# Two-path attention with two feed-forward layers on one core: band tiles of 26 queries by 32 keys in place of 58 by 64

## The reference

```
q_d, k_d, v_d = means over groups of 4 positions           # 144 rows each
out_up   = repeat(softmax(q_d k_d^T / 8) v_d, 4)            # the average path
scores   = q k^T / 8, where |i - j| < 4, else -1e9          # the band path: 7 keys a query
out_local = softmax(scores) v
x = out_up + out_local                                      # then (2304 tokens, 512)
x = (h * sigmoid(h)) @ w_out,        h = x @ w_in           # layer 1, 512 -> 2048 -> 512
x = (h * sigmoid(1.702 h)) @ w_out,  h = x @ w_in           # layer 2
```

## Time and profile before

| | |
|---|---|
| median of three runs | 809.04 us (807.85 to 809.33) |
| profiled execution | 808.21 us, span 806.4 us |
| TensorE, VectorE, ScalarE, GpSimd busy in the span | 98%, 80%, 66%, 26% |
| attention | from 5.3 us to 106.7 us |
| granted TensorE clock | full in every slice |

### The profile page before, as it was taken

One profiled execution on the slowest core, in us unless ns is written; L12 is line 12 of the kernel. 1 busy time (PEld: TensorE's weight loads), 2 busy tenths in 40 slices (PEclk: granted clock), 3 DMA queues, 4 the chain that ended last, 5 costly groups with the idle time before them and its releaser, 6 DMA issues.

```text
span 806.4 us, 15771 instructions
## 1 busy us (share of the span) xinstructions
PE 790.0 (98%) x5864; PEld 763.4 (95%) x5864; DVE 646.0 (80%) x905; ACT 530.8 (66%) x849; POOL 208.8 (26%) x203
## 2 busy tenths in 40 slices
PE   9888799999999999999999999999999999999998
PEld 5666599999999999999999999999999999999998
DVE  7999899999898778998678898899555688456466
ACT  5878865677655678555687556678455786465673
POOL 5899977520274220445200000000000000000000
PEclk9999999999999999999999999999999999999999
DMA  8877647787878887677877778868887877878773
GB/s 282 266 249 238 197 150 259 262 298 233 283 236 268 260 315 245 217 261 258 289 267 249 239 250 262 256 224 272 306 275 257 273 249 266 304 250 271 264 256 136
DMA packets 100763, 205.51 MB, mean 255 GB/s; under 512 B 8784, under 2 KB 56400, under 8 KB 100688
## 3 DMA queue, kind: packets, MB, share of 16 engines
q1 hardware_dynamic: 100688, 204.51, 76.0%
HBM read 160.96 MB, written 43.52 MB: 254 GB/s over the span
## 4 chain that ended last, share of the span: by engine, by line
PE 88%; POOL 8%; issue 3%; DVE 1%; ACT 0%; POOLq 0%; DVEq 0%
PE hid L351 43%; PE yp L377 42%; POOL vpair L1038 2%; POOL vavg L1042 1%; PE yp L393 1%; POOL pband L1032 1%; POOL G L1062 1%; POOL G L1063 1%; POOL G L1068 1%; POOL G L1066 1%; POOL x L284 0%; DVE wh L315 0%; PE sc L1342 0%; PE hp L1342 0%; PE pt L1229 0%
## 5 line engine op out<-in xcount | busy, mean ns | idle before, releaser
L351 PE MATMUL hid<-xs,wh 128*128 128x384 f32 x2016 | 351.3, 334 | 0.7 <-issue 0.4
L351 PEld LDWEIGHTS hid<-xs,wh 128*128 128x128 f32 x2016 | 349.3, 188 | 1.7 <-issue 1.4
L377 PE MATMUL yp<-gr,wh 128*128 128x384 f32 x1968 | 342.1, 334 | 0.0
L377 PEld LDWEIGHTS yp<-gr,wh 128*128 128x128 f32 x1968 | 341.2, 188 | 0.1
L306 ACT ACTIVATE wh<-wr 128x1024 fp32r<-128x1024 f32 (+1 forms) x164 | 164.6, 1004 | 149.8 <-PE hid L351 120.0
L569 DVE TENSOR_TENSOR gr<-G,gr 128x768 fp32r<-128x768 f32 x144 | 137.9, 964 | 52.7 <-ACT gr L449 52.7
L449 ACT ACTIVATE gr<-G 128x768 fp32r<-128x768 f32 x144 | 121.8, 845 | 66.9 <-PE yp L377 66.8
L315 DVE TENSOR_TENSOR wh<-wr,wh 128x1024 fp32r<-128x1024 f32 x76 | 95.1, 1251 | 19.0 <-ACT wh L306 18.8
L412 ACT ACTIVATE G<-G 128x1152 f32<-128x1152 f32 x48 | 55.7, 1161 | 0.8 <-DVE G L564 0.8
L533 DVE TENSOR_TENSOR hv<-p,hid 128x384 f32<-128x384 f32 x48 | 26.3, 548 | 29.8 <-PE hid L351 28.0
L559 DVE TENSOR_TENSOR G<-hv,hid 128x384 f32<-128x384 f32 x48 | 26.3, 549 | 28.2 <-PE hid L351 28.2
(11 more groups left out here) (101 smaller groups left out, 748.0 us busy)
## 6 DMA issues: line engine op xcount, KB each, us to landing
wh<-rests SPq DMA_DIRECT2D x72, 512.0 KB, 3.7
wr<-sums_out SPq DMA_DIRECT2D x48, 512.0 KB, 4.7
wr<-in_w_out SPq DMA_DIRECT2D x36, 512.0 KB, 5.2
rests<-wh SPq DMA_DIRECT2D x36, 512.0 KB, 3.5
wr<-sums_in SPq DMA_DIRECT2D x40, 384.0 KB, 4.0
wr<-in_w_in SPq DMA_DIRECT2D x40, 256.0 KB, 3.5
qk<-in_qkT SPq DMA_DIRECT2D x11, 576.0 KB, 4.8
G<-in_w_in SPq DMA_DIRECT2D x12, 512.0 KB, 5.3
```

The lines of the kernel that those rows point to most:

```text
L351: last = eng.matmul(hid[:, at, 0:HALF], lhsT=wh[:, w % SLOTS, part, a % 4, cc * P:(cc + 1) * P], rhs=xs[:, rest, q, cc, :], start=start an ...
L377: last = eng.matmul(yp[:, at + m, 0:HALF], lhsT=wh[:, w % SLOTS, part, p % 4, m * P:(m + 1) * P], rhs=gr[:, p, rest, :], start=start and p ...
```

## The change

22 tiles of 26 queries and 32 keys take the place of the 10 (the first and the last have 28 queries). In `scores` a slot is now 32 columns wide and holds four tiles, one on each 32 rows; 12 slots, 384 columns, head 0 in the first 192 and head 1 in the other 192, each in its own half of `sc`. The tiles of each head form two parts of 11.

- Scores: 44 matmuls (2 heads x 22 tiles), weights 64 features by 32 queries, 32 moving columns; for each tile head 0, then head 1. The outer tiles are no exception any more, and the wait on `half_sc` is gone.
- Mask: two bf16 products of 192 columns. It is made by more steps: GpSimd fills `band4` and `ends` and cuts them with six affine selects, VectorE takes a maximum over four (new semaphore `band_max`), and ScalarE copies in three steps.
- VectorE's three passes and ScalarE's exponential go over 12 slots of 32 columns (33 with a guard); GpSimd's multiplication writes to a tile of its own, `probs`, in another order, so VectorE's subtraction has a new wait on `b_nrm` of two units back.
- Transposes: three of 128x128 in one group, where there were five in two; one copy of 384 columns where there were two. There are three groups a unit in place of four.
- Band products: 44 matmuls, weights 32 keys by 64 features, 26 moving columns (28 at the ends). The keys of (head, part) = (0,0), (0,1), (1,0), (1,1) lie on rows 0, 32, 64 and 96 onwards. Part 0 writes the first half of `po`, part 1 the second; head h writes output rows 64h onwards. `vwin` holds 11 windows of 64 features on each row, where it had 5 of 128.

```diff
-    QT = 64
-    WIN = 64
-    NT = 10
-    HALF = NT // 2
+    QT = 32
+    WIN = 32
+    PART = 11
+    NT = 2 * PART
+    SLOTS, BLOCKS = 12, 3
     NQ = WIN - 2 * (FACTOR - 1)
-    FIRST_Q = S - (NT - 1) * NQ
-    q0 = [max(0, FIRST_Q + NQ * (t - 1)) for t in range(NT)]
-    nq = [FIRST_Q] + [NQ] * (NT - 1)
+    nq = [NQ + 2] + (NT - 2) * [NQ] + [NQ + 2]
+    q0 = [sum(nq[:t]) for t in range(NT)]
     starts = [min(max(q - (FACTOR - 1), 0), S - WIN) for q in q0]
-    SLOT_TILES = ((1, 2), (5, 6), (3, 4), (7, 8))
-    def place(h, t):
-        if t in (0, NT - 1):
-            return 4 + t // (NT - 1), h
-        k = [t in two for two in SLOT_TILES].index(True)
-        return 6 * h + k, SLOT_TILES[k].index(t)
+    def place(r, i):
+        return 3 * r + i // 4, slice(i % 4 * QT, (i % 4 + 1) * QT)
...
-    SC = 512 - HALF * WIN
+    SC = 512 - SLOTS // 2 * WIN
     REST = SD - P
     NA = 3
     AQ = SD // NA
-    AR = QT + AQ
-    GROUPS = ((0, 3), (3, 5))
-    NLG = len(GROUPS)
-    NG = NLG + 2
-    FREED = (0, -2, -1, 1)
+    AR = D + AQ
+    NG = 3
+    FREED = (-2, -1, 0)
...
-            pband = [sb(f"pband{i}", [P, HALF, 2 * WIN + 2]) for i in range(2)]
-            probs = [t[:, :, 1:2 * WIN + 1] for t in pband]
-            mxb, smb, rcb = (sb(n, [P, NT]) for n in ("mxb", "smb", "rcb"))
+            pband = [sb(f"pband{i}", [P, SLOTS, WIN + 1]) for i in range(2)]
+            probs = [sb(f"probs{i}", [P, BLOCKS, 4, WIN]) for i in range(2)]
+            mxb, smb, rcb = (sb(n, [P, SLOTS]) for n in ("mxb", "smb", "rcb"))
...
-            scores = sc[:].rearrange("p a n -> p (a n)")[:, SC:SC + NT * WIN]
+            scores = sc[:].rearrange("p a n -> p (a n)")[:, SC:SC + SLOTS * WIN]
...
-                for h in range(2):
-                    part = band3[h * QT:(h + 1) * QT]
-                    eng.affine_select(out=part, in_=part, compare_op=ALU.is_ge, fill=NEG, base=FACTOR - 1,
-                                      pattern=[[-sign * (FACTOR - 1), 3], [sign, WIN]],
-                                      channel_multiplier=-sign).then_inc(consts_fill, 1)
+                for part, before, places in ((band4[:], FACTOR - 1, [[-sign * QT, 4]]), (ends[0:QT, 0, :], 0, []),
+                                             (ends[2 * QT:3 * QT, 1, :], FACTOR, [])):
+                    eng.affine_select(out=part, in_=part, compare_op=ALU.is_ge, fill=NEG,
+                                      base=FACTOR - 1 + sign * before, pattern=places + [[-sign, WIN]],
+                                      channel_multiplier=sign).then_inc(consts_fill, 1)
...
-                e = probs[u.odd].rearrange("p b (s n) -> p b s n", n=WIN)
-                eng.tensor_tensor(e, e, rcb[:].rearrange("p (b s) -> p b s", s=2).unsqueeze(3).broadcast_to(e.shape),
+                to = probs[u.odd][:]
+                eng.tensor_tensor(to, pband[u.odd][:, :, 0:WIN].rearrange("p (r b) n -> p b r n", b=BLOCKS),
+                                  rcb[:].rearrange("p (r b) -> p b r", b=BLOCKS).unsqueeze(3).broadcast_to(to.shape),
                                   ALU.mult).then_inc(b_nrm, 1)
...
-            eng.wait_ge(consts, 1)
-            slots = band[:].rearrange("p (g s) n -> p g s n", g=2)
-            eng.activation(slots[:, :, 0:4, :], band3[:, 1:2, :].unsqueeze(1).broadcast_to([P, 2, 4, WIN]),
+            eng.wait_ge(band_max, 1)
+            eng.activation(band[:, 1:, :], band[:, 0:1, :].broadcast_to([P, SLOTS // 2 - 1, WIN]),
                            ACT.Copy).then_inc(band_cp, 1)
-            eng.activation(band[:, 4:6, :], band3[:, 0:3:2, :], ACT.Copy).then_inc(band_cp, 1)
+            eng.wait_ge(band_cp, 1)
+            eng.activation(band[0:QT, 0, :], ends[0:QT, 0, :], ACT.Copy).then_inc(band_cp, 1)
+            eng.activation(band[2 * QT:3 * QT, SLOTS // 2 - 1, :], ends[2 * QT:3 * QT, 1, :],
+                           ACT.Copy).then_inc(band_cp, 1)
...
-                    e = probs[u.odd].rearrange("p b (s n) -> p b s n", n=WIN)
-                    eng.wait_ge(band_sc, 2 * (u.n + 1))
-                    eng.tensor_reduce(mxb[:], scores.rearrange("p (t n) -> p t n", n=WIN), AX.X,
-                                      ALU.max).then_inc(b_max, 1)
+                    e, tiles = pband[u.odd][:, :, 0:WIN], scores.rearrange("p (t n) -> p t n", n=WIN)
+                    eng.wait_ge(band_sc, u.n + 1)
+                    eng.tensor_reduce(mxb[:], tiles, AX.X, ALU.max).then_inc(b_max, 1)
                     eng.wait_ge(b_max, u.n + 1)
-                    eng.tensor_tensor(e, scores.rearrange("p (b s n) -> p b s n", s=2, n=WIN),
-                                      mxb[:].rearrange("p (b s) -> p b s", s=2).unsqueeze(3).broadcast_to(e.shape),
+                    if u.n > 1:
+                        eng.wait_ge(b_nrm, u.n - 1)
+                    eng.tensor_tensor(e, tiles, mxb[:].unsqueeze(2).broadcast_to(e.shape),
                                       ALU.subtract).then_inc(b_sub, 1)
...
+            eng.wait_ge(consts, 1)
+            eng.tensor_reduce(band[:, 0, :], band4[:].rearrange("p g n -> p n g"), AX.X, ALU.max).then_inc(band_max, 1)
...
-                for a in (0, HALF):
-                    eng.matmul(scores[:, a * WIN:(a + HALF) * WIN], lhsT=ident16[:],
-                               rhs=band[:, a:a + HALF, :].rearrange("p t n -> p (t n)"),
+                for h in range(2):
+                    eng.matmul(scores[:, h * SLOTS // 2 * WIN:(h + 1) * SLOTS // 2 * WIN], lhsT=ident16[:],
+                               rhs=band[:].rearrange("p t n -> p (t n)"),
                                start=True, stop=False, skip_group_check=True)
                 flat = qk[u.n % 3].rearrange("p i s -> p (i s)")
-                def head_scores(h, t):
-                    (slot, side), rows = place(h, t), slice(h * D, (h + 1) * D)
-                    return eng.matmul(scores[side * QT:(side + 1) * QT, slot * WIN:(slot + 1) * WIN],
-                                      lhsT=flat[rows, q0[t]:q0[t] + QT], rhs=flat[rows, S + starts[t]:S + starts[t] + WIN],
-                                      start=False, stop=t in (0, NT - 1), skip_group_check=True)
-                for two in SLOT_TILES:
-                    for h in range(2):
-                        for t in two:
-                            last = head_scores(h, t)
-                last.then_inc(half_sc, 1)
-                head_scores(0, 0)
-                head_scores(1, NT - 1)
-                eng.wait_ge(half_sc, u.n + 1)
-                head_scores(1, 0).then_inc(band_sc, 1)
-                head_scores(0, NT - 1).then_inc(band_sc, 1)
+                for part in range(2):
+                    for i in range(PART):
+                        for h in range(2):
+                            t, rows = part * PART + i, slice(h * D, (h + 1) * D)
+                            slot, to = place(2 * h + part, i)
+                            last = eng.matmul(scores[to, slot * WIN:(slot + 1) * WIN], lhsT=flat[rows, q0[t]:q0[t] + QT],
+                                              rhs=flat[rows, S + starts[t]:S + starts[t] + WIN],
+                                              start=False, stop=t == NT - 1, skip_group_check=True)
+                last.then_inc(band_sc, 1)
...
-                    for i in range(a, b):
-                        last = transpose(to[:, (i - a) * P:(i - a + 1) * P], probs[u.odd][:, i])
+                eng.wait_ge(*((a_nrm, NA * (u.n + 1)) if j else (b_nrm, u.n + 1)))
+                if j == 0:
+                    for b in range(BLOCKS):
+                        last = transpose(to[:, b * P:(b + 1) * P], probs[u.odd][:, b].rearrange("p r n -> p (r n)"))
...
-                for two in ((1, 5), (2, 6), (3, 7), (4, 8), (0, 9)):
-                    for t in two:
-                        low = t // HALF * WIN
-                        for h in range(2):
-                            slot, side = place(h, t)
-                            last = eng.matmul(po[h * D:(h + 1) * D, PO + q0[t]:PO + q0[t] + nq[t]],
-                                              lhsT=vwin[low:low + WIN, u.odd, t % HALF, h * D:(h + 1) * D],
-                                              rhs=ptb[low:low + WIN, slot // 2, side * QT:side * QT + nq[t]],
-                                              start=True, stop=True)
+                for i in range(PART):
+                    for r in range(4):
+                        (slot, side), keys, h, t = place(r, i), slice(r * WIN, (r + 1) * WIN), r // 2, r % 2 * PART + i
+                        last = eng.matmul(po[h * D:(h + 1) * D, PO + q0[t]:PO + q0[t] + nq[t]],
+                                          lhsT=vwin[keys, u.odd, i, :], rhs=ptb[keys, slot % 3, side][:, 0:nq[t]],
+                                          start=True, stop=True)
                 last.then_inc(band_out, 1)
...
```

(37 more changed lines are left out.)

34 lines of the change are left out of this document (15 added, 19 removed).

## The result

The changed kernel takes 833.54 us (median of 4 runs, 831.58 to 834.97); the kernel before, run beside it, 808.99 (807.85 to 809.33). The ratio is 1.0304, 95% interval 1.0280 to 1.0328. The forecast of 830.7 us is nearly met, and its range holds the time. The mechanism it gave is not what happened: the number came out right for the wrong reason. Two runs far above the rest, one of the kernel before (2738 us) and one of experiment 11 (1573 us), are left out of the ratios.

The account below looks back on a forecast made before the run. VectorE and GpSimd set the attention's pace; TensorE would become the bound. Fourteen units +17.9 us, first two +2.1, last +1.7: +21.7 on 808.2 gives 829.9, median 0.8 above: 830.7 us, range 825 to 836.

Parts of the forecast that it names:

- The cheaper passes: Attention unit: fewer columns save VectorE 0.75 us over three passes, GpSimd 0.33, TensorE's mask and transposes 0.34.
- a weight load on other rows waits for the one in front: TensorE's scores and band products: all 88 matmuls of a unit go one at a time, costing +0.54 and +1.96 us.
- two matmuls a step: Old kernel's band products: each 0.058 us step was read as two matmuls with two records each.
- Unit 7.33 throughout, no alternation, no gap: Attention: TensorE's unit lasts 7.33 us mask to mask, never alternating, with no TensorE wait on GpSimd or ScalarE.
- Rival 3: Row groups overlap two at a time: products +0.74, scores -0.15, TensorE's unit 5.4 us, kernel 804 us; chance 0.09.
- Rival 4: Matmuls overlap four at a time, products in 11 steps: TensorE's unit 4.7 us, kernel 800.5 us; chance 0.09.
- the forecast's own sign: Attention: a unit of 5.1 to 5.9 us would say that a rival with a faster kernel holds.
- ScalarE's wait covered, `b_nrm` free, the mask's new steps: TensorE's ScalarE wait hidden by longer products; VectorE's new `b_nrm` wait free; extra mask steps nothing, at most 0.5 us.
- The end +1.7: Last attention unit's transposes and products, beside the feed-forward part's first group: -0.23 and +1.96, together +1.7 us.
- Afterwards nothing: Feed-forward part after the attention: no change, as TensorE is at 100% there.
- The rule on halves: Skill page: different row tiles cannot access one PSUM bank at once, so new products go at most two at a time.
- +17.9 us of work: Attention's 14 steady units at 7.33 us each: 102.6 us against 84.7 before.

Follow-up runs that it names:

- experiment 11: Kernel before the change, with GpSimd's normalisation of the probabilities done three times a unit in place of once; 851.82 us, ratio 1.0524.
- experiment 1: Changed kernel with its 44 band products reordered, all 11 tiles of one 32-row group and then the next group; 899.98 us, ratio 1.1119.
- 2: Changed kernel with the band products in two passes, row groups 0 and 1 in turn, then 2 and 3; 840.74 us (one run).
- experiment 3: Kernel before the change, with 48 small f32 matmuls more a unit, all on one place of the array; 863.04 us, ratio 1.0664.
- 4: Kernel before the change, with 48 small f32 matmuls more a unit, spread over four places of the array; 834.25 us, ratio 1.0317.
- 5: Changed kernel with one unused 512 KB copy within DRAM more in each attention unit, on SyncE's queue; 844.55 us, ratio 1.0444.

## Why the prediction was right in its number and wrong in its reason

- **The cheaper passes: right.** Forecast 0.25 us for each of VectorE's three; the maximum fell from 815 to 557 ns, the sum from 825 to 555. GpSimd's step fell by 0.41 (0.33 forecast), mask and transposes by 0.10 and 0.22 (0.11 and 0.23). The groups of the changed kernel, against the earlier trace rows:

```profile
L1031 POOL TENSOR_TENSOR probs<-pband,rcb 128x384 f32<-128x384 f32 x15 | 12.8, 851 | 37.8 <-DVE rcb L1182 37.7
...
L1164 DVE TENSOR_REDUCE mxb<-sc 128x12 f32<-128x384 f32 x14 | 7.8, 557 | 12.2 <-PE sc L1250 11.9
```

- **The failed step: "a weight load on other rows waits for the one in front".** Products were forecast at +1.96 us a unit and cost +0.67 (1.48 less 0.81); scores at +0.54 and cost -0.15. The narrow windows of a product block (all columns as in the earlier trace rows) show four records begun within 0.05 us, as in the kernel before, and 84 by 1.25 us:

```profile
80.50:80.55 0.05, 0.04 (x4) 0.04 (x4) 1.00 0.00 0
80.50:81.75 1.25, 1.24 (x84) 1.24 (x87) 1.00 0.66 185
```

  The forecast took four records in one step for two matmuls with two records each. The first two records of this block (80.510 to 80.522 us) have 28 and 26 moving columns, so they belong to different matmuls:

```profile
L1289 PE MATMUL po<-yt,vwin x2: 233/234/235, 80.5 to 80.5; 32*64 32x28 f32 x1, 32*64 32x26 f32 x1
```

  The first four go 28, 26, 28, 26, and the next four, 79 ns behind them, 28, 26, 28, 26 again: a step is four matmuls on four places, one record of each, and their second records are the next step. The old products went through four places too (two row halves by two output halves), with the same spacing (6 to 7 ns within a group of four, 58 from group to group), so 40 records took 10 x 0.058. I took "two matmuls a step" for a limit of pairs, though it was the hold time of a record shared out over four places; experiments 1 and 2 (58 ns, then half, then a quarter) show it. By this reading the products cost 48 records more x 14.5 ns = 0.70, and TensorE's unit is 5.17 - 0.11 - 0.23 + 0.67 - 0.15 = 5.35; it is 5.28.
- **"Unit 7.33 throughout, no alternation, no gap": wrong.** Units take from 5.28 to 10.45 us. Rival 3 had the amount of work right (products +0.74 and scores -0.15 forecast, +0.67 and -0.15 measured; TensorE 5.4, measured 5.28), though not its reason. Rival 4 had the manner, four at a time, but counted 11 steps where 88 records make 22, so its 4.7 is too low. By either the kernel would have been faster; the forecast's own sign for that, a unit of 5.1 to 5.9 us, came true in the undisturbed units, and the kernel is slower all the same. No rival had the two costs that decided: instructions that come too late, and the clock that falls. The earlier trace rows held the first one's size (1588 matmul records in the 14 units, to which the change adds 14 x 94 = 1316), and nothing in them its price.
- **ScalarE's wait covered, `b_nrm` free, the mask's new steps: nearly right.** One wait for ScalarE is left (0.85 us); the third mask begins 0.6 us later, not 2.1.
- **The end +1.7: 2.3, for another reason** (gaps of 3.6 us, less the shorter work). **Afterwards nothing: right.** From 129.66 to the end of the span are 700.1 us, before 699.7.
- **The rule on halves.** The products of row groups 0 and 2 write the same half of `po`, and so do 1 and 3, yet the four start within 20 ns and a record costs 14.5 ns. The Trainium skill, "TensorEngine Tiling (Array Packing)", Restrictions and Gotchas, would allow two at a time at most; for these short products the trace does not agree. The Trainium skill, "TensorEngine Tiling (Array Packing)", Key Properties, says that different tiles can load and multiply in parallel; the prediction held this contradicted, and the trace agrees with it. The averages' scores (144 columns, both heads into one half) take as long as before, 0.94 us for 12 records. The prediction read "no two overlap" there and saw the rule in it. Their records start in pairs 6 to 7 ns apart, one pair each 122 ns or more. As on one place no two records start less than 31 ns apart (experiment 3), a pair is probably one record of each head, side by side in one half. That was argued and not tried.

That the sum met the time is coincidence: +17.9 us of work that doesn't exist stand for 12.2 of gaps and 15.8 of low clock, less 8.7 gained.

**What is shown, what is open.** Shown: four places run in parallel; gaps end with the arrival of instructions (1.2 to 1.7 us after a packet, all 113), come with the instruction rate (3 against 4) and grow with other traffic (5); idle time lowers the clock (11), and so do small matmuls on one place without any (1). Not shown: how much of the changed kernel's half clock is due to each of the two. Some of its gaps (1.66 and 1.80 us, at 48.50 and 116.92) were followed by no fall, while its longest stretch at half (13.6 us, from 23.55) came after gaps of 1.16 and 0.63. None of the kernels is faster than the one before by more than the noise.

## What to carry to other kernels

Cutting matmuls into smaller tiles that run side by side saves TensorE time only as long as its instructions can be brought: count records (two a matmul in f32, and as many weight loads) per us before and after, not only their durations. Look for "issue" gaps inside runs of equal matmuls and at the granted clock of each stretch; a short gap may cost as much again in the clock. And read the price of a small matmul as the time for which it holds its place, divided by the places in turn.

## What the runs showed of the hardware

- A f32 matmul record holds its place 58 ns with 64 weight columns and 26 to 58 moving ones (after, before, experiment 1), 31 to 32 ns with 32 weight columns and 8 moving ones (experiment 3); over different places records follow each other at 14.5 ns (products), and (0.96 - 0.22) / 87 = 8.5 ns (scores).
- Instructions come in packets of 16.4 KB (0.97 MB in 59). The gaps of the changed kernel lie 124 to 127 matmul records apart, or a multiple of that; 1504 records more made 12 packets more, 125 each. A gap ends 1.20 to 1.68 us after a packet does (113 gaps in 11 kernels), and no two packets of an attention start less than 3.31 us apart in any run.
- The clock was at half for 119.5 us in an attention in which TensorE had 0.3 us of gaps (experiment 1), and for 6.2 us after a wait of 3.05 us (experiment 11).
